# GpSimd takes the third pair's sums after C21's split, ScalarE rounds that pair, and w_out's pair goes ahead of w_in's sums

## The reference, cut to what matters

```python
kv  = einsum('bhsd,bhse->bhde', k, v)          # batch 4, 8 heads, 576 tokens, head_dim 64
out = einsum('bhsd,bhde->bhse', q, kv)
x   = out / sqrt(mean(out*out, -1) + 1e-6) * g_norm     # then 2304 tokens x 512
h = x @ w_in1;  x = (h * sigmoid(1.702 * h)) @ w_out1   # 512 -> 2048 -> 512
h = x @ w_in2;  x = softplus(h) @ w_out2                # 512 -> 2048 -> 512
```

## Time and profile before

| | us |
|---|---|
| median of 3 runs | 817.43 |
| lowest and highest | 816.87 and 817.56 |
| the profiled execution, its own time | 818.9 |
| its span, first to last instruction | 817.1 |
| mean granted TensorE clock | 0.998 of full speed |

### The profile page before, as it was taken

How to read it: one execution, slowest core, us unless ns; L and a number is a source line. 1 busy time by engine, 2 the same in 40 slices (tenths; PEclk the granted TensorE clock), 3 DMA queues, 4 the chain that set the end, 5 groups by cost and what they waited for, 6 DMA issues and landing times.

```text
span 817.1 us, 12401 instructions
## 1 busy us (share of the span) xinstructions
PE 806.3 (99%) x4614; PEld 735.5 (90%) x4614; DVE 587.0 (72%) x1029; ACT 424.8 (52%) x809; POOL 224.5 (27%) x263
## 2 busy tenths in 40 slices
PE   8998999999999999999999999999999999999998
PEld 7887999999999999999998888898988988989886
DVE  3788767687665686665678777888767889766774
ACT  4772332334221233222246776688767678766765
POOL 4889887304422403263501401200000000000000
PEclk9999999999999999999999999999999999999999
DMA  9955536435455472756543535324433323452402
GB/s 357 406 191 186 229 143 267 172 116 206 163 224 180 164 249 91 241 200 254 228 161 114 206 100 205 109 90 148 167 124 117 154 91 99 159 181 90 147 35 78
DMA packets 24427, 139.80 MB, mean 171 GB/s; under 512 B 2224, under 2 KB 6960, under 8 KB 17200
## 3 DMA queue, kind: packets, MB, share of 16 engines
q1 hardware_dynamic: 24224, 138.95, 46.3%
q10 hardware_dynamic: 144, 0.07, 0.0%
HBM read 104.92 MB, written 34.08 MB: 170 GB/s over the span
## 4 chain that ended last, share of the span: by engine, by line
PE 91%; DVE 4%; DMA 2%; ACT 1%; issue 1%; SPq 0%; ACTq 0%; DVEq 0%
PE ps L660 42%; PE ps L728 24%; PE ps L736 15%; PE ps L733 8%; DMA kv_in_sb<-k_v 2%; DVE xs_f L1015 1%; DVE gs_f L1083 1%; DVE gs_f L1044 0%; DVE rms L984 0%; PE ps L601 0%; DVE gs L1097 0%; DVE gs L1093 0%; PE ps L584 0%; DVE ex L1106 0%; ACT rms L791 0%
## 5 line engine op out<-in xcount | busy, mean ns | idle before, releaser
L660 PE MATMUL ps<-xs,w_in 128*128 128x384 f32 x2016 | 410.3, 339 | 2.6 <-DVE gs_f L1044 2.3
L660 PEld LDWEIGHTS ps<-xs,w_in 128*128 128x128 f32 x2016 | 357.7, 188 | 27.5 <-DVE gs_f L1044 3.8
L728 PE MATMUL ps<-w_out,gs 128*128 128x512 f32 x864 | 226.1, 393 | 0.0
L1044 DVE TENSOR_TENSOR gs_f<-ps,gs_f 128x384 f32<-128x384 f32 x240 | 133.1, 555 | 115.9 <-PE ps L660 114.4
L728 PEld LDWEIGHTS ps<-w_out,gs 128*128 128x128 f32 x864 | 160.0, 188 | 24.1 <-issue 0.5
L736 PE MATMUL ps<-gs,w_out 128*128 128x512 f32 x576 | 148.7, 393 | 0.0
L736 PEld LDWEIGHTS ps<-gs,w_out 128*128 128x128 f32 x576 | 105.9, 188 | 16.4
L835 ACT ACTIVATE lg<-gs_f 128x384 f32<-128x384 f32 x73 | 38.3, 525 | 128.3 <-DVE gs_f L1044 127.6
L505 POOL TENSOR_TENSOR w_in<-w_in_f,w_in 128x256 fp32r<-128x256 f32 x112 | 95.3, 886 | 28.5 <-ACT w_in L877 28.2
L733 PE MATMUL ps<-gs,w_out 128*128 128x256 f32 x576 | 83.6, 281 | 0.9 <-issue 0.9
L872 ACT CAST gs<-gs_f 128x384 fp32r<-128x384 f32 x96 | 48.9, 509 | 67.7 <-DVE gs_f L1113 66.5
(11 more groups left out here) (64 smaller groups left out, 588.2 us busy)
## 6 DMA issues: line engine op xcount, KB each, us to landing
w_in<-w_kept SPq DMA_DIRECT2D x40, 1792.0 KB, 7.3
w_kept<-w_in SPq DMA_DIRECT2D x16, 1792.0 KB, 10.2
w_in_f<-w_in SPq DMA_DIRECT2D x16, 512.0 KB, 4.0
w_out_f<-w_out SPq DMA_DIRECT2D x16, 512.0 KB, 8.7
kv_in_sb<-k_v SPq DMA_DIRECT2D x8, 640.0 KB, 10.9
kv_in_sb<-k_v SPq DMA_DIRECT2D x8, 576.0 KB, 12.6
q_sb<-q_t SPq DMA_DIRECT2D x16, 288.0 KB, 11.0
out<-xy SPq DMA_DIRECT2D x18, 256.0 KB, 7.7
```

Of the source, the lines that this page charges most:

```text
L660: mm = nc.tensor.matmul(ps[:, bank, 0:HALF], w[:, wp, W_OF[k], cols], xs[:, k, xp, t], start=(new and t == 0 and (wp, xp) == (HI, HI)), st ...
L728: mm = nc.tensor.matmul(ps[:, acc_bank(1, j), 0:DM], g[:, j * P:(j + 1) * P], w, start=new, stop=done)
L1044: nc.vector.tensor_tensor(to, bank, other, ALU.add).then_inc(added, 1)
```

## The change

`W_POOL` goes from 3 to 2, so that the pairs 0 and 1 of w_in are rounded by GpSimd and pair 2 by ScalarE; `w_low(d)` now waits for the (d - 1)th rounding. GpSimd makes the sums of pair 2 behind the wait for C21's split instead of ahead of it. In the steps 1 to 5 GpSimd does w_out_low(m) ahead of w_sums(m + 2). ScalarE does round_w_in(2) in step 1 behind C11's sigmoid and ahead of round_w_out(1); round_w_in(3) moves from step 1 (between C22's and C12's sigmoid) to step 2, behind round_w_out(2); round_w_in(4) to round_w_in(7), in the steps 2 to 5, move from behind round_w_out(m) to between C22's and C12's sigmoid.

```diff
-    W_POOL = 3
+    W_POOL = 2
...
             w_out_low(0, 0)
+            pool.wait_ge(g_split, C21 + 1)
             w_sums(2)
-            pool.wait_ge(g_split, C21 + 1)
-            w_high(2)
+            pool.wait_ge(w_hi_made, 1)
             w_low(2)
             for m in range(1, ALL):
                 d = split_at(m)
...
+                if m < STEPS - 2:
+                    for pair, layer in w_out_of(m):
+                        w_out_low(pair, layer)
                 if d:
                     w_sums(d)
-                for pair, layer in w_out_of(m):
-                    w_out_low(pair, layer)
+                if m >= STEPS - 2:
+                    for pair, layer in w_out_of(m):
+                        w_out_low(pair, layer)
                 if d:
                     pool.wait_ge(w_hi_made, d - W_POOL + 1)
                     w_low(d)
...
-            LATE_ROUNDS = (1, STEPS)
+            LATE_ROUNDS = (2, 3, 4, 5, STEPS)
...
                 if m > 0:
                     hidden(m, C11)
+                if m == 1:
+                    round_w_in(2)
                 if m > 0:
                     for pair, layer in w_out_of(m):
                         round_w_out(pair, layer)
-                if split_at(m) and m not in LATE_ROUNDS:
+                if split_at(m) and m not in (0, 1) + LATE_ROUNDS:
                     round_w_in(split_at(m))
+                if m == 2:
+                    round_w_in(3)
```

## The result

The changed kernel takes 820.36 us (median of 7 runs, 819.85 to 820.48) where the kernel before takes 817.43 (median of 7, 816.87 to 818.33). The ratio is 1.0031, 95% interval 1.0021 to 1.0041: slower by 0.3%. A second set, with 12 and 17 runs, gave 820.66 against 818.53, ratio 1.0026 (1.0017 to 1.0034). The forecast was 818.3, with "within 0.2%" as the likeliest case and 0.25 for slower. The measured median lies 0.2 us above the stated range of 815.8 to 820.2; 817.43 times the ratio is 820.0.

A forecast was written before the change was run, and what follows sets the result against it. TensorE, busy 99%, lost 4.8 us around steps 0 to 1 to waits on VectorE and slow clock. The sum -4.8 + 0.55 + 0.5 + 3.0 + 1.6 = +0.85 on 817.43 gave 818.3 us, range 815.8 to 820.2.

The forecast's parts named there:

- within 0.2%: Whole kernel: step 1's gain is real but given back at step 3, -1.05 to +1.6 us; chance 0.63.
- step 1, against the profile before: Step 1: later w_sums(2) and the cast on ScalarE remove two TensorE waits and the slow clock, gain 4.8 us.
- wait for w_out_low(1): Down product of step 1 waits for GpSimd's w_out_low(1), done at 75.8: cost 0.55 us (0 to 0.9).
- wait for w_out_low(2): Down product behind P1 of step 3 waits for w_out_low(2), done at 92.1: cost 0.5 us (0 to 0.9).
- P2 of step 3 waits for first_product(3): Step 3: ScalarE's copy, queued behind pair 4's late cast, holds up TensorE: cost 3.0 us (2.5 to 3.5).
- low clock and U2 behind it: Step 3, behind P2's wait: TensorE waits for U2 or runs at low clock: cost 1.6 us (0.95 to 2.0).
- ScalarE's stand: Step 2: ScalarE stands from about 87.6 to 95.2 us for w_sums(4), before rounding pair 4.
- R: Step 2: the time when ScalarE finishes rounding pair 4 (round_w_in(4)), forecast at 96.9 us.
- carries over: Whole kernel: the profiled execution's 1.5 us over the median stays as an offset, giving a median of 818.3.
- The second (the gain is kept): Steps 2 and 3: ScalarE's stand is covered, giving 813.7 to 814.7 us; chance 0.12.
- The third in its form: The clock falls also for the 0.5 us waits at 75.2 and 91.5, each adding 1.7 us: 820.0 or 821.7; chance 0.13.
- The fourth: P4 of step 1: VectorE stays the bound, 0.9 us less gain, or 819.1 to 820.8 if the clock falls; chance 0.12.

The follow-up runs named there:

- after's second profile: The changed kernel unedited, measured and profiled again beside runs of the kernel before: 820.66 us (12 runs), ratio 1.0026.
- the second profile of before: The kernel before, unedited, measured and profiled once more: 817.62 us (10 runs), ratio 0.9993, span of the profile 815.6.
- the halves of w_out_low(1): Changed kernel with pair 4's sums in step 1, plus w_out_low(1) split around w_low(2) and ScalarE's rounds reordered: 815.62 us, ratio 0.9965.
- the rest of the change: The kernel before with the change's other GpSimd and ScalarE moves, pair 2's sums and cast left as before: 822.48 us, ratio 1.0057.
- the cast alone: The kernel before with only pair 2's rounding moved from GpSimd to ScalarE, GpSimd's order as before: 816.56 us, ratio 0.9975.
- the one without: Pair 2's cast alone on ScalarE, plus w_out_low(1) ahead of w_sums(3) in step 1 and casts of pairs 3, 4 moved: 815.35 us, ratio 0.9965.

## Why the prediction was right, and where it was off

**The mechanism** was as forecast, step by step. In the table, the excess of each stretch over a clean step of 15.73 or 15.74 us, from the first pair of profiled executions.

| term | predicted | measured |
|---|---|---|
| step 1, against the profile before | -4.8 | -4.73 (17.06 against 21.79 to P1 of step 2) |
| wait for w_out_low(1) | 0.55 | 1.04 (16.78 - 15.74) |
| wait for w_out_low(2) | 0.5 | 0.54 (0.43, and 0.11 in the matmuls behind it) |
| P2 of step 3 waits for first_product(3) | 3.0 | 2.79 (98.07 against 95.28) |
| low clock and U2 behind it | 1.6 | 1.87 (13.71 against 11.84) |
| sum | +0.85 | +1.51 |

The last three are one stretch, P1 of step 3 to P1 of step 4, 20.93 us or 5.20 over a clean step. The low clock varies: with after's second profile the last term is 2.92 (14.76 against 11.84), outside the 0.95 to 2.0 that the prediction gave it. ScalarE's stand (7.89 us, 7.6 predicted) and R (97.2, 96.9 predicted) came out as worked out, and so did the price of nothing from step 4 on and for the DMAs.

**What failed** is one step, in two places of the text: "an idle stretch of 1.87 us was followed by 3.4 us of half clock", taken as part of every execution of before, and with it the sentence that the 1.5 us between the profiled execution and the median "carries over". It does not. Without the low clock before loses 3.2 us in step 1 and not 4.8: P1 of step 2 lies 17.06 us from the start in after and 77.37 - 57.11 = 20.26 in the second profile of before. Of the 2.1 us that the prediction put down to slow clock in step 1, 1.5 was; the rest is there at full clock too (3.2 lost, with waits of 2.73). Against that execution the change costs 54.77 - 51.73 = 3.04 us, and the medians of the first measurement above differ by 2.93; that compares after with its usual fall and before without one. With 3.2 in place of 4.8 the prediction's own sum gives +2.45, or 819.9. A profile 1.5 us over the median of its own kernel should have been read as holding an event that the median execution has not.

**Luck.** That the range held is owed to the room left at its upper end for the rivals 3 and 4, neither of which happened in the form described. The outcome called likeliest, within 0.2%, did not come: the change is slower by 0.3%.

**A smaller miss** is the wait for w_out_low(1), priced at 0.55 and measured at 1.04: the four instructions took 3.87 us and not 3.31 beside VectorE's gates of C21 and C22, and TensorE's matmuls behind the wait take 0.1 us more (1.33 against 1.23). The bound of 0.9 was set too low.

**The rivals.** The second (the gain is kept) did not happen, and the changed kernel with pair 4's sums moved, with and without the halves of w_out_low(1), shows what it would have been worth: 815.6 to 815.8 us. The third in its form (a fall behind the waits of 0.5 us) is not in any profile: after waits of 0.79, 0.97 and 0.28 us the clock stayed at 1.00. The clock did matter in another way: it fell behind the 2.62 us wait in both profiles of after, once for twice as long, though not behind 2.63 us in the profile of the rest of the change. The fourth is out: P4 of step 1 did not wait.

**The parts of the change.** Of the 3.2 us that pair 2's part gains in step 1 at full clock (20.26 to 17.06 us from the start to P1 of step 2), the cast alone gives 2.2 (18.10). Holding the sums back until C21 is split gives the other 1.0, the 0.87 us wait; but then w_low(2) begins 9.33 us behind the start (66.34 - 57.01) instead of 6.68 (63.37 - 56.69), and no version with it beat the one without; between 815.35 and 815.62, measured in the same set, no difference is shown. That GpSimd's order in the steps 3 to 5 (w_out first, casts between C22's and C12's sigmoid) costs nothing was seen in the traces and not tried by itself.

## What to carry to other kernels

When a wait is put into an in-order queue, follow the queue until the engine that waits has caught up: here a cast moved by one step made GpSimd late, the next cast stood 7.9 us for GpSimd, and the sigmoid and copy behind it stopped TensorE some 14 us behind the moved cast (81.57 to 95.45 us). The debt of a busy helper engine (12.5 us of work in a 15.7 us step, and 1.4 us made up) moved on until a stop of TensorE paid for it, and the cure here was work in the gap where the helper itself waited. And when a profiled execution is off the median of its kernel, find out what in that profile is not in the others before any of its stretches is counted as gain.

## What the hardware showed that was not expected

- The low clock is an event of some executions. With the same program and the same wait of 1.87 us, it fell to 0.50 for 3.4 us in one profile and not at all in another. Runs of before with a mean clock of 0.998 or less are 9 of 23 (and 1 of 10), 6 of 10 and 10 of 17 in the three sets of experiments; of after, 6 of 7 and 10 of 12. Behind after's wait of 2.62 us it fell for about 3.4 us in one profile and 6.8 in the other, and behind 2.63 us in the profile of the rest of the change not at all. Behind waits of 0.28 to 0.97 us it fell in no profile. What decides it is not shown. Before's two groups of runs lie 1.4 us apart (818.97 against 817.52).
- A VectorE product of two SBUF operands takes 0.54 us beside an idle GpSimd, 0.85 to 1.09 beside its sums, and 1.84 beside its 1.68 us cast; taking that one cast off GpSimd freed a whole gate, 1.3 us in the product alone.
